# Attention and two feed-forward layers on one core: four TensorE runs a pair in place of eight

## What is computed

```python
scores = scale * np.matmul(q, k.transpose(0, 1, 3, 2))      # B, H, S, D = 4, 8, 576, 64, causal mask
a = np.exp(scores - scores.max(-1, keepdims=True))
a /= a.sum(-1, keepdims=True) + 1e-09
local = np.matmul(a, v)
q_p = phi(q)                                                # elu(q) + 1
mem_out = einsum(q_p, M_prev) / (einsum(q_p, z_prev) + 1e-06)
x = g * mem_out + (1 - g) * local                           # g = sigmoid(beta), one number a head
x = (silu(x @ w_gate) * (x @ w_val)) @ w_out                # 2304 tokens, 512 -> 1536 -> 512
out = g2(x @ w_in) @ w_out2                                 # 512 -> 2048 -> 512, g2 a clipped square
```

## Time and profile before

| | us |
|---|---|
| median of 3 runs (982.23 to 983.0) | 982.42 |
| the profiled execution | 983.68 |
| its span in the profile | 981.9 |
| TensorE busy (share of the span) | 967.0 (98%) |
| VectorE busy | 704.1 (72%) |
| ScalarE busy | 463.7 (47%) |
| GpSimd busy | 305.1 (31%) |
| first product of the feed-forward part starts at | 182.64 |

### The profile page before, as it was taken

How to read it: one execution, slowest core, us unless ns; L and a number is a source line. 1 busy time by engine, 2 the same in 40 slices (tenths; PEclk the granted TensorE clock), 3 DMA queues, 4 the chain that set the end, 5 groups by cost and what they waited for, 6 DMA issues and landing times.

```text
span 981.9 us, 18870 instructions
## 1 busy us (share of the span) xinstructions
PE 967.0 (98%) x6372; PEld 926.6 (94%) x6372; DVE 704.1 (72%) x1369; ACT 463.7 (47%) x940; POOL 305.1 (31%) x291
## 2 busy tenths in 40 slices
PE   8999999999999999999999999999999999999998
PEld 7777777999999999999999999999999999999998
DVE  6888989577777555557555568888886777867766
ACT  6899999655445223234222336544543334433331
POOL 5777776166672000100001156575310010000000
PEclk9999999999999999999999999999999999999999
DMA  7554543389878655555555534767775744538321
GB/s 247 166 160 150 170 146 106 122 302 339 321 268 333 244 193 208 223 222 214 217 194 193 207 124 179 251 232 274 277 262 194 286 170 184 208 147 298 138 106 65
DMA packets 46156, 204.72 MB, mean 209 GB/s; under 512 B 5488, under 2 KB 5872, under 8 KB 46064
## 3 DMA queue, kind: packets, MB, share of 16 engines
q1 hardware_dynamic: 45920, 203.52, 56.9%
q10 hardware_dynamic: 144, 0.00, 0.0%
HBM read 147.33 MB, written 56.17 MB: 207 GB/s over the span
## 4 chain that ended last, share of the span: by engine, by line
PE 86%; ACT 5%; issue 3%; DVE 3%; DMA 2%; POOL 1%; SPq 0%; ACTq 0%; DVEq 0%; POOLq 0%
PE ps L1454 25%; PE ps L1455 24%; PE ps L1456 24%; PE ps L1425 5%; PE ps L1368 5%; ACT pt L809 3%; PE ps L1398 3%; DMA kept_ul<-wu_l 1%; DVE xt_l L1109 1%; ACT tmp L919 0%; PE ps L1344 0%; DMA wu_r<-w_up 0%; DVE xy L1224 0%; ACT xt_h L840 0%; DVE negs L1048 0%
## 5 line engine op out<-in xcount | busy, mean ns | idle before, releaser
L1454 PE MATMUL ps<-xt_h,wu_h 128*128 128x384 f32 x840 | 281.4, 335 | 2.7 <-ACT u2s L889 1.7
L1456 PE MATMUL ps<-xt_h,wu_l 128*128 128x384 f32 x840 | 280.8, 334 | 0.0
L1455 PE MATMUL ps<-xt_l,wu_h 128*128 128x384 f32 x840 | 280.8, 334 | 0.0
L1454 PE MATMUL ps<-hid_h,wd_h 128*128 128x384 f32 x672 | 225.5, 336 | 2.9 <-DVE xy L1224 2.4
L1455 PE MATMUL ps<-hid_l,wd_h 128*128 128x384 f32 x672 | 224.6, 334 | 0.0
L1456 PE MATMUL ps<-hid_h,wd_l 128*128 128x384 f32 x672 | 224.6, 334 | 0.0
L1224 DVE TENSOR_TENSOR xy<-xy,ps 128x384 f32<-128x384 f32 x288 | 158.6, 551 | 69.9 <-PE ps L1456 69.1
L904 ACT ACTIVATE hid_h<-hid_r 128x768 fp32r<-128x768 f32 x84 | 70.7, 842 | 201.7 <-DVE hid_r L1198 139.7
L1454 PEld LDWEIGHTS ps<-xt_h,wu_h 128*128 128x128 f32 x840 | 157.7, 188 | 4.6 <-issue 3.5
L1455 PEld LDWEIGHTS ps<-xt_l,wu_h 128*128 128x128 f32 x840 | 157.7, 188 | 0.0
L1456 PEld LDWEIGHTS ps<-xt_h,wu_l 128*128 128x128 f32 x840 | 157.7, 188 | 0.0
(11 more groups left out here) (87 smaller groups left out, 1282.4 us busy)
## 6 DMA issues: line engine op xcount, KB each, us to landing
wu_l<-kept_ul SPq DMA_DIRECT2D x40, 896.0 KB, 7.5
wu_h<-kept_uh SPq DMA_DIRECT2D x40, 896.0 KB, 5.2
kept_uh<-wu_h SPq DMA_DIRECT2D x20, 896.0 KB, 6.8
kept_ul<-wu_l SPq DMA_DIRECT2D x20, 896.0 KB, 8.5
wd_h<-kept_dh SPq DMA_DIRECT2D x28, 512.0 KB, 3.7
wd_l<-kept_dl SPq DMA_DIRECT2D x28, 512.0 KB, 4.7
wu_r<-w_up SPq DMA_DIRECT2D x20, 512.0 KB, 5.1
qk<-qk_in SPq DMA_DIRECT2D x15, 640.0 KB, 4.9
```

Of the source, the lines that this page charges most:

```text
L1454: nc.tensor.matmul(dst, w_hi, v_hi, start=start, stop=False, skip_group_check=onto)
L1455: nc.tensor.matmul(dst, w_hi, v_lo, start=False, stop=False, skip_group_check=onto)
L1456: return nc.tensor.matmul(dst, w_lo, v_hi, start=False, stop=stop, skip_group_check=onto)
```

## The change

TensorE's step now has four stretches: the scores of tile 4; all nine turns of the preceding pair, with the first block's scores ahead of the last of them; the scores of tiles 3, 2 and 1; the values of the preceding pair, in the order of tiles 2, 1, 4, 3. The nine groups are turned in a new order with new banks. Copies (3, 1) and (2, 1) go from ACT to DVE and (2, 0) from DVE to ACT, so that ACT has six copies and DVE three. Bank 7, whose part of `out_x` is now multiplied first, holds the third group turned, (3, 0). The other engines' loops follow: on POOL `v_scale(p)`, which stood in step p + 1, comes first in step p, ahead of the four `mem_rows` of that step and of the feed-forward preparations; `phi_z` and `relu_q` (now two pairs ahead) come last. DVE's `out_x` of two pairs back follows `sums_inverse`. ACT's `exp_q` comes first. SP's program is unchanged.

```diff
-        ON_DVE = ((4, 1), (2, 0))
-        BANK = {(4, 0): 4, (4, 1): 5, (4, 2): 4, (3, 0): 5, (3, 1): 6, (2, 0): 7, (2, 1): 4, (1, 0): 5, (1, 1): 4}
+        TURNS = ((4, 0), (4, 1), (3, 0), (4, 2), (3, 1), (2, 0), (1, 0), (2, 1), (1, 1))
+        ON_ACT = ((4, 0), (3, 0), (4, 2), (2, 0), (1, 0), (1, 1))
+        ON_DVE = ((4, 1), (3, 1), (2, 1))
+        BANK = {(4, 0): 4, (4, 1): 5, (4, 2): 6, (3, 0): 7, (3, 1): 4, (2, 0): 5, (2, 1): 6, (1, 0): 7, (1, 1): 5}
+        VALUES = (2, 1, 4, 3)
...
 @block.gpsimd
-            for p in range(NPAIR + 1):
+            relu_q(1)
+            for p in range(NPAIR):
                 j = SLOTS * p
                 if p > 0:
-                    mem_rows(j - 1)
-                    v_scale(p - 1)
-                if p + 1 < NPAIR:
-                    relu_q(p + 1)
-                if p < NPAIR:
-                    mem_rows(j)
+                    v_scale(p)
...
-                    mem_rows(j + 1)
-                    mem_rows(j + 2)
+                for k in range(SLOTS):
+                    mem_rows(j + k)
                 if p + 1 < NPAIR:
                     phi_z(p + 1)
+                if p + 2 < NPAIR:
+                    relu_q(p + 2)
...
 @block.scalar
+                if 0 < p < NPAIR - 1:
+                    exp_q(p + 1)
                 if p > 0:
-                    copy_pt(j - SLOTS, (2,))
-                    for k in range(1, SLOTS):
-                        copy_pt(j - SLOTS + k, (0, 1))
+                    for i, g in ON_ACT[:-1]:
+                        copy_pt(p - 1, i, g)
                 if p < NPAIR:
                     exp_tile(j)
...
+                if p > 0:
+                    copy_pt(p - 1, *ON_ACT[-1])
                 if p < NPAIR:
-                    exp_tile(j + 1)
-                    exp_tile(j + 2)
-                    copy_pt(j, (0, 1))
-                    exp_tile(j + 3)
+                    for k in range(1, SLOTS):
+                        exp_tile(j + k)
...
 @block.vector
+                if 0 < p <= NPAIR:
+                    sums_inverse(p - 1)
                 if p > 1:
+                    out_x(p - 2, 1)
                     out_x(p - 2, 0)
-                    out_x(p - 2, 1)
...
 @block.tensor
-                if group_bank(j, g) >= 6: at_least(pe, x_done, 2 * (p - 1) + group_bank(j, g) - 5)
+                if group_bank(j, g) == 7: at_least(pe, x_done, 2 * p - 1)
+                if group_bank(j, g) == 6: at_least(pe, x_done, 2 * p)
...
                 if p < NPAIR:
                     scores(SLOTS * p)
                 if p > 0:
-                    turn(SLOTS * (p - 1), (2,))
-                    for k in range(1, SLOTS):
-                        turn(SLOTS * (p - 1) + k, (0, 1))
+                    for i, g in TURNS[:-1]:
+                        turn(p - 1, i, g)
                 if p < NPAIR:
                     scores_f(p)
                 if p > 0:
-                    values(SLOTS * (p - 1))
+                    turn(p - 1, *TURNS[-1])
                 if p < NPAIR:
                     for k in range(1, SLOTS):
                         scores(SLOTS * p + k)
-                    turn(SLOTS * p, (0, 1))
                 if p > 0:
-                    for k in range(1, SLOTS):
-                        values(SLOTS * (p - 1) + k)
+                    for i in VALUES:
+                        values(p - 1, i)
```

More of the change, by code:

```diff
@@ L395, in group_at @@
[L395 to L407, removed]
@@ new lines, in attention_two_ffns, with turned_count, turned_all @@
+        VALUES = (2, 1, 4, 3)
+        def turned_count(j, g):
+            p, i = tile_of(j)
+            return len(TURNS) * p + TURNS.index((i, g)) + 1
+        def turned_all(j):
+            return max(turned_count(j, g) for g in range(len(GROUPS[tile_of(j)[1]])))
+        def copied(j, g):
+            p, i = tile_of(j)
+            if (i, g) in ON_DVE:
+                return pt_dve, len(ON_DVE) * p + ON_DVE.index((i, g)) + 1
+            return pt_act, len(ON_ACT) * p + ON_ACT.index((i, g)) + 1
@@ L417, in group_bank, with values_count, step_of, copied_under @@
+        def values_count(j):
+            p, i = tile_of(j)
+            return SLOTS * p + VALUES.index(i) + 1
+        def step_of(p, i):
+            return SLOTS * p + SLOTS - i
         def group_bank(j, g):
             return BANK[tile_of(j)[1], g]
[L422 to L427, removed]
+        def copied_under(j, g):
+            p, i = tile_of(j)
+            before = [x for x in TURNS[:TURNS.index((i, g))] if BANK[x] == BANK[i, g]]
+            if before:
+                return copied(step_of(p, before[-1][0]), before[-1][1])
+            if p == 0:
+                return None
+            last = [x for x in TURNS if BANK[x] == BANK[i, g]][-1]
+            return copied(step_of(p - 1, last[0]), last[1])
@@ L429, in chunk_col, with copied_last @@
+        def copied_last(p, bank):
+            last = [x for x in TURNS if BANK[x] == bank][-1]
+            return copied(step_of(p, last[0]), last[1])
         def chunk_col(i, n):
@@ L795, in exp_tile, with copy_pt @@
                                          accum_out=rsum[:, p % 2, 0:1]).then_inc(expdf, 1)
[L797 to L809, removed]
+            def copy_pt(p, i, g):
+                j = step_of(p, i)
+                if j >= PTS:
+                    act.wait_ge(pv_done, values_count(j - PTS))
+                act.wait_ge(turned, turned_count(j, g))
+                if ends_pair(j, g):
+                    at_least(act, r_out, 32 * (p - 1))
+                    nc.scalar.activation(rrow[0:NBLK, p % 2], r_rows(j), ACT.Copy).then_inc(r_row, 1)
+                dst, src = group_ends(j, g)
+                nc.scalar.activation(dst, src, ACT.Copy).then_inc(pt_act, 1)
             def up_high(u, n):
@@ L1405, in values @@
-            def values(j):
-                p, i = tile_of(j)
+                if copied_under(j, g):
+                    pe.wait_ge(*copied_under(j, g))
+                if group_bank(j, g) == 7:
+                    at_least(pe, x_done, 2 * p - 1)
+                if group_bank(j, g) == 6:
+                    at_least(pe, x_done, 2 * p)
+                a, b = GROUPS[i][g]
+                for c in range(a, b):
+                    col = chunk_col(i, c)
+                    mm = nc.tensor.transpose(ps[:, group_bank(j, g), (c - a) * P:(c - a + 1) * P],
+                                             rown[:, j % ROWN, col:col + P], ident[:])
@@ L1414, in values @@
-                if i == 2:
-                    at_least(pe, x_done, 2 * p)
+                at_least(pe, v_scaled, p + 1)
+                at_least(pe, x_done, 2 * p - (bank == 7))
+                pe.wait_ge(*copied_last(p, bank))
                 for g in range(len(GROUPS[i])):
```

129 lines of the change are left out of this document (55 added, 74 removed).

## The result

| | before | changed |
|---|---|---|
| median, us | 982.51 (982.23 to 983.65, 6 runs) | 986.12 (984.96 to 987.75, 6 runs) |
| ratio, 95% interval | | 1.0033 (1.0022 to 1.0043) |
| span of the profiled execution | 981.9 | 983.2 |
| first product of the feed-forward part | 182.64 | 185.11 |

The account below looks back on a forecast made before the run. TensorE was taken to bound the attention part, others having little room. Step 1 -1.1, steps 2-7 -2.9, 8-13 -0.5, 14 -0.6, 15 -0.6, last stretch +0.8: together -4.9, from 982.42 to 977.5 us, range 973.3 to 983.2.

Parts of the forecast that it names:

- TensorE's part: TensorE's passes and surcharges in an attention step: 9.92 us, with a 0.1 wait 10.02 at best, where 10.69 was measured before.
- The reciprocals' ring: From the reciprocals' copy through `rbc` and `out_x` to group (3, 0): 10.1 us a step, 10.47 with the mean wait.
- GpSimd's ring: V's load, scaling, `mem_rows`, `phi_z`, next load's issue: 8.6 us, with preparations 10.1 in steps 2-7, 10.5 in 8-13.
- the term for the four `mem_rows`: GpSimd's four `mem_rows` in its ring: 0.36 from each start to the next instruction, 0.1 for a wait, about 1.85 us.
- the light: Steps 2 to 7, with two small preparations on GpSimd: four at 10.1 us, two at 10.4, together -2.9.
- heavy steps: Steps 8 to 13, with one preparation of 1.83 us on GpSimd: taken at 10.6 each, together -0.5.
- VectorE's busy time holds waits inside instructions: Why VectorE's 10.1 us a step was not taken to exceed the bound of 10.02; the cover was called thin.
- Rival D: V's landing grows in GpSimd's ring, 1 us per us: at a landing of 4.5, +5.9, 988 us; chance 0.12.
- steps 8 to 13 over 11 mean C or D: Sign in the attention timeline: steps 8 to 13 exceeding 11 us mean Rival C or Rival D; V's landing tells which.
- Rival C: Reciprocals' write held until V's load has landed: ring 11.2 us, steps 8 to 13 give back 3.6, 981.1; chance 0.21.
- Step 14: Attention step with no load ahead of V's: forecast to gain 0.6 us.
- The last stretch: After pair 15's scores: eight more turns +0.87, reciprocals' return +0.3, surcharges -0.36: together +0.8 us.

Follow-up runs that it names:

- e1: Changed kernel with GpSimd scaling V of the preceding pair, v_scale(p - 1), first in step p, as before the change: 979.45 us.
- e2: Changed kernel with SP issuing load_v(p) before load_nat(p + 2), so V's load no longer waits for phi_z: 979.14 us.
- e4: Changed kernel with GpSimd's v_scale as a one-input tensor_scalar with factor 1.0, leaving out the scaling of V: 992.47 us.
- e3: Changed kernel with rnorm_q on VectorE moved ahead of tile 3's maxima, before GpSimd's scaling of V: 987.09 us.
- e11: Changed kernel with the edits of e2 (V's load issued first) and e5 (first block's scores behind the last turn): 977.76 us.
- e7: Changed kernel with the copy of group (3, 1) moved back from VectorE to ScalarE: 987.66 us.
- e10: Changed kernel with VectorE's splitting moved to right behind rnorm_q: 987.3 us.
- e5: e1 with the first block's scores on TensorE placed behind the last turn instead of ahead of it: 979.13 us.

## Why the prediction was wrong

- **TensorE's part** was right in kind, and 0.3 too small in size. In e1, where nothing else holds it, the even steps are 10.33, against a floor of 10.02. Scores of tiles 3 to 1 and the values came out to 0.1 of the working. The stretch from tile 4's scores to those of tile 3 is longer: 24 turns take 101.44 - 98.61 = 2.83 in e1, where 0.06 + 24 x 0.109 gives 2.68, and the piece around the first block's scores costs another 0.16, which went when they moved behind the last turn.
- **The reciprocals' ring** did not set the steps: in the changed kernel VectorE waited for `rbc` once between 10 and 176 us, for 0.4.
- **GpSimd's ring** was named, with its members on GpSimd and SP in their place, and is what slowed the kernel (e2: two lines exchanged on SP, 7 us). The step that failed is its sum: the term for the four `mem_rows`, "about 1.85", is 2.0 to 2.9 in the light and 2.6 to 2.85 in the heavy steps, and the two preparations, "which I estimate at 0.75 each", take 1.4 to 2.1 together. Undisturbed, neither is over the forecast: 1.54 (e4, steps 3 to 7) and 1.38 (step 7). Two things were left out. `phi` and the splitting on VectorE and the preparations and `mem_rows` on GpSimd meet, and stand still for one another; that is all of the excess in the heavy steps. And `mem_rows` wait for `mem_scale`, which makes VectorE a member of the ring; that is most of the excess in steps 2 to 5. It too hangs on the standstill: with the norms moved out of its way (e3), no step of the ring has such a wait. So most light steps became 10.7 to 10.8, no shorter than before's 10.69, and most heavy ones 10.9 to 11.6. The two stretches missed by 2.6 and 2.9: 5.5 of the 7.4 us by which the first product did.
- **"VectorE's busy time holds waits inside instructions"** was seen, and the earlier trace rows used to say that there was room. What those waits wait for was not asked, though before had the pair of rows at 101.46 and 101.83.
- **Rival D**, the slower one, had the right ring and price, but the wrong term: the landing stayed at 3.5 in the median. The prediction's sign, that steps 8 to 13 over 11 mean C or D, was met by steps 10 to 13 and means neither.
- **Rival C**: its mechanism is there, and costs next to nothing in the changed kernel, because the reciprocals have room in a ring of 10.8 (below).
- Step 14 took 11.37 and not 10.09. In e1, e2 and e11, without the ring, it is still 10.8, so the ring is at most 0.6 of this miss; the rest is open, with the 10.8 of steps 12 to 14. The last stretch, forecast at 17.9 us after pair 15's scores, took 18.5 here and 18.3 to 19.0 in those three, so its estimate was too small by itself; which part of it isn't shown.

## What to carry to other kernels

When a step is put first in an engine's loop, ask what issues its load, and whether that issue waits for the end of the same loop: then the whole loop is one ring, and one line in the DMA queue's order can open it. Add such a ring up from rows in which its members run beside what they will run beside. A VectorE instruction that lasts many times as long as its like is a wait: look for GpSimd's two-input instruction that ends with it, and expect that moving one of the two can move the wait rather than remove it.

## What the runs showed of the hardware

**The standstill**, with its sizes: norms 0.17 to 1.16, `mem_scale` 0.15 to 1.77; GpSimd's own instructions 1.26 to 1.78 and 1.82 to 2.52. With one SBUF input on GpSimd there is none: `mem_scale` in e4, above, and in the kernel before norms and splitting beside `relu_q`:

```profile
104.58 1.65 POOL L642 TENSOR_SCALAR qrelu<-nat 128x576 f32<-128x576 f32 x1
...
105.66 0.17 DVE L1033 SCALAR_TENSOR_TENSOR norms<-norm,gt 128x9 f32<-128x9 f32 x1
```

**Late loads.** Of the changed kernel's 12 loads in the ring all landed within 3.7 us. In the profiles of e3, e4, e7 and e10 one to five land only after 4.0 to 5.3, and each lengthens its ring. Why they are late isn't shown, nor whether such loads make the 1.1 us that the changed kernel's profile doesn't place.

**A write that counts late.** The Trainium skill, DMA: Bandwidth & Descriptors, section Queues, rings and completion order, has a transfer's semaphore rise only after earlier writes of its DMA engine. In the changed kernel's step 9 (rows above) V's load is issued at 103.83, and GpSimd starts on it at 107.26; the reciprocals' write and read there:

```profile
104.51 0.68 SPq L517 DMA_DIRECT2D rsums<-rrow  x1
...
107.39 1.13 SPq L526 DMA_DIRECT2D rbc<-rsums  x2
```

and in e2, where V's load was issued 4.60 ahead of the write:

```profile
102.60 0.67 SPq L517 DMA_DIRECT2D rsums<-rrow  x1
...
104.95 1.13 SPq L526 DMA_DIRECT2D rbc<-rsums  x2
```

2.88 against 2.35. Over the changed kernel's steps 5 to 13 the load is issued 0.5 to 1.0 ahead of the write, and the read follows the write after 2.9 to 3.6; before, 1.5 to 1.7 ahead, after 2.35 to 2.40 in 11 of 12. In seven of the nine steps the read leaves within 0.4 of V's landing. The traces agree with the rule, and e5's slow step 7 fits it. There V's load was issued 1.20 ahead of the write and landed only after 4.5, at 73.47, and the read left 0.13 later:

```profile
68.92 0.43 SPq L511 DMA_DIRECT2D vm<-vm_in  x1
...
70.12 0.69 SPq L517 DMA_DIRECT2D rsums<-rrow  x1
...
73.60 1.13 SPq L526 DMA_DIRECT2D rbc<-rsums  x2
```

One row of e5 doesn't fit so simply: behind the write at 29.41 the read left at 31.81, 1.0 ahead of the landing of V's load. The rule is for one DMA engine, and no trace here shows on which of them the late part of that load ran.
